# Orders of ScalarE's and VectorE's work in the first and last steps of an attention loop

## The reference

```python
# q, k, v: (4, 8, 576, 64); s: (4, 8, 576)
scores = scale * q @ k^T                                  # scale = 1/8
cum    = cumsum(max(s, 0))
scores = where(causal, -1e9, scores + minimum(-(cum[q] - cum[k]), 0))
attn   = exp(scores - max); attn /= sum(attn) + 1e-9
x      = (attn @ v), heads side by side                   # (2304, 512)
h = x @ w_in; x = (h - tanh(h)) @ w_out                   # 512 -> 2048 -> 512
h = x @ w2_in; solu = h * softmax(h); x = layernorm(solu) * g @ w2_out   # 512 -> 1024 -> 512
```

## Time and profile before

| | before |
|---|---|
| median of 3 runs | 807.65 us (807.53 to 807.90) |
| the profiled execution | 807.74 us |
| its span (first to last instruction) | 805.9 us |
| TensorE matmul busy | 796.3 us, 99% |
| ScalarE busy | 396.0 us, 49% |
| VectorE busy | 465.2 us, 58% |
| GpSimd busy | 274.3 us, 34% |

### The profile page before, as it was taken

How to read it: one execution, slowest core, us unless ns; L and a number is a source line. 1 busy time by engine, 2 the same in 40 slices (tenths; PEclk the granted TensorE clock), 3 DMA queues, 4 the chain that set the end, 5 groups by cost and what they waited for, 6 DMA issues and landing times.

```text
span 805.9 us, 14646 instructions
## 1 busy us (share of the span) xinstructions
PE 796.3 (99%) x4532; PEld 670.5 (83%) x4532; DVE 465.2 (58%) x1099; ACT 396.0 (49%) x936; POOL 274.3 (34%) x323
## 2 busy tenths in 40 slices
PE   8999999999999999999999999999999999999998
PEld 7788888888888899988888888888888888888886
DVE  5889999897954342432233222453568766666661
ACT  5999999998543232322223222442435434433342
POOL 3778877878100000000000000016553755444400
PEclk9999999999999999999999999999999999999999
DMA  6655566554523200000000000002000000000001
GB/s 174 171 151 150 143 153 161 149 144 119 159 93 103 79 1 1 1 1 1 1 0 0 0 0 0 1 1 99 6 1 0 27 27 27 26 26 13 26 13 53
DMA packets 77723, 46.40 MB, mean 58 GB/s; under 512 B 59824, under 2 KB 68144, under 8 KB 77680
## 3 DMA queue, kind: packets, MB, share of 16 engines
q1 hardware_dynamic: 75232, 45.19, 20.1%
q10 hardware_dynamic: 2448, 0.66, 0.4%
HBM read 40.97 MB, written 4.87 MB: 57 GB/s over the span
## 4 chain that ended last, share of the span: by engine, by line
PE 93%; POOL 2%; issue 2%; DVE 1%; DMA 1%; ACT 1%; POOLq 0%; DVEq 0%; ACTq 0%; SPq 0%
PE psum L1490 25%; PE psum L1477 24%; PE psum L1760 11%; PE psum L1727 11%; PE psum L1579 7%; PE psum L1612 5%; PE psum L1536 5%; PE psum L1743 2%; PE psum L1630 2%; PE psum L1554 1%; PE psum L1540 1%; DMA cum_bc<-cum_dram 1%; POOL x_lo L677 0%; ACT probs L894 0%; DMA cum_dram<-probs 0%
## 5 line engine op out<-in xcount | busy, mean ns | idle before, releaser
L1477 PE MATMUL psum<-x_hi,w1i 128*128 128x512 f32 (+1 forms) x640 | 182.1, 369 | 0.0
L1490 PE MATMUL psum<-gate_hi,w1o 128*128 128x512 f32 (+1 forms) x640 | 146.0, 370 | 0.0
L1477 PEld LDWEIGHTS psum<-x_hi,w1i 128*128 128x128 f32 x640 | 115.5, 188 | 20.5 <-DVE w1i L1129 0.4
L1490 PEld LDWEIGHTS psum<-gate_hi,w1o 128*128 128x128 f32 x640 | 112.5, 188 | 21.1
L1172 DVE TENSOR_TENSOR gate_lo<-gate,gate_hi 128x512 fp32r<-128x512 f32 (+1 forms) x80 | 53.5, 669 | 125.2 <-ACT gate_hi L869 125.2
L1477 PE MATMUL psum<-x_lo,w1i 128*128 128x512 f32 (+1 forms) x320 | 117.8, 368 | 0.0
L711 POOL TENSOR_TENSOR w2t<-stage 128x512 f32<-128x512 f32 x2 | 4.3, 2159 | 327.9 <-DVE w2x L1146 327.9
L869 ACT ACTIVATE gate_hi<-gate 128x512 fp32r<-128x512 f32 (+1 forms) x80 | 47.2, 590 | 134.9 <-PE psum L1490 126.5
L1160 DVE TENSOR_TENSOR gate<-psum,gate 128x512 f32<-128x512 f32 (+1 forms) x80 | 51.0, 638 | 95.8 <-ACT gate L856 94.3
L856 ACT ACTIVATE gate<-psum 128x512 f32<-128x512 f32 (+1 forms) x80 | 44.5, 556 | 111.7 <-PE psum L1477 90.7
L894 ACT ACTIVATE probs<-probs,neg_max 128x128 f32<-128x128 f32 (+2 forms) x144 | 83.6, 586 | 9.6 <-DVE neg_max L1205 9.6
(11 more groups left out here) (159 smaller groups left out, 1411.3 us busy)
## 6 DMA issues: line engine op xcount, KB each, us to landing
cum_bc<-cum_dram SPq DMA_DIRECT2D x16, 576.0 KB, 5.0
rden_T<-rden_dram SPq DMA_DIRECT2D x32, 144.0 KB, 3.1
out_x<-out_sb SPq DMA_DIRECT2D x18, 256.0 KB, 2.0
stage<-in_q SPq DMA_DIRECT2D x32, 128.0 KB, 2.5
v_raw<-in_v SPq DMA_DIRECT2D x32, 128.0 KB, 3.8
stage<-in_moe_w_in SPq DMA_DIRECT2D x16, 256.0 KB, 2.9
stage<-in_moe_w_out SPq DMA_DIRECT2D x16, 256.0 KB, 3.1
stage<-in_k SPq DMA_DIRECT2D x28, 128.0 KB, 2.4
```

What stands on the lines that cost most here:

```text
L1477: mm = pe.matmul(h_ps[j % 4][:, 0:wide(c)], wp[j][:, kt, :], xp[:, kt, 0:wide(c)], start=(n == 0), stop=(n == 3 * KT - 1))
L1490: mm = pe.matmul(y_ps[m][:, 0:wide(c)], wp[j][:, m * P:(m + 1) * P], gp[j % 2][:, 0:wide(c)], start=(j == 0 and wp is w1o_hi and gp is gat ...
```

## The change

In words:

- Step 0: ScalarE's third copy (k of pair 1) goes ahead of exp(0, 2), VectorE's third low part ahead of bias(0, 3). The tail's exponential of pair 0 moves from the end of step 0 into step 1.
- Step 1, ScalarE: an order of its own. A01 first, then the tail's exponential of pair 0, A2, copy 0, the denominators of pair 0, A3, copy 1, exp(0, 0), T, and the other exponentials behind it; B3 ahead of exp(1, 3). ScalarE's copy of k (`qk_copy(2)`) is left out; VectorE makes it (`k_copy`), behind A3's low part. VectorE makes A2's low part before the reciprocals.
- Step 15: ScalarE copies x's second half and T before exp(0, 2), not after it; GpSimd scales x before the last block of `first_x` and the high part of v; the denominators of pair 15 move into step 16, behind the copy of x's first half.
- The first up product waits block by block for x's high part, and for the low part only at the matmul that reads it.

```diff
--- before.py
+++ after.py
@@ -686,9 +686,12 @@
                     pool.wait_ge(w1i_hi_done, 1)
                     pool.tensor_tensor(w1i_lo[0][:, :, :], stage[0][:, 0:BANK].rearrange("p (k f) -> p k f", k=KT),
                                        w1i_hi[0][:, :, :].bitcast(F32), ALU.subtract).then_inc(w1i_first_done, 1)
+                    scale_x()
                     first_x(3)
-                v_hi()
-                scale_x()
+                    v_hi()
+                else:
+                    v_hi()
+                    scale_x()
                 v_lo()
 
             pool.wait_ge(pool_const, 11)
@@ -885,7 +888,7 @@
                             hi = act.activation(to(pT_hi), ps, ACT.Copy)
                         hi.then_inc(p_hi_done, 1)
 
-                def exp(h, t):
+                def exp(h, t, sl=sl):
 
                     if sl.runs(0):
                         pair, half, par = sl.pair(0)
@@ -939,44 +942,62 @@
                     for h in range(2):
                         exp(h, 0)
                         exp(h, 1)
-                    qk_copy(0)
-                    qk_copy(1)
+                    for n in range(3):
+                        qk_copy(n)
                     exp(0, 2)
-                    qk_copy(2)
                     exp(1, 2)
                     exp(0, 3)
                     exp(1, 3)
+                    return
+                if sl.fixed and sl.s == 1:
+
+                    p_hi("A01")
+                    exp(None, FULL, Slot(0, 0, PAIRS))
+                    p_hi("A2")
+                    qk_copy(0)
+                    denominators(Slot(0, 0, PAIRS))
+                    p_hi("A3")
+                    qk_copy(1)
+                    exp(0, 0)
+                    p_hi("T")
+                    rden_rows_copy()
+                    exp(0, 1)
+                    exp(1, 0)
+                    exp(1, 1)
+                    exp(0, 2)
+                    p_hi("B01")
+                    exp(1, 2)
+                    p_hi("B2")
+                    exp(0, 3)
+                    p_hi("B3")
+                    exp(1, 3)
                     exp(None, FULL)
+                    denominators()
                     return
-
-                second = sl.fixed and sl.s == 1
                 x_low_part(0)
+                if sl.fixed and sl.s == PAIRS:
+                    denominators(Slot((PAIRS - 1) // 2, (PAIRS - 1) % 2, PAIRS))
                 p_hi("A01")
                 exp(0, 0)
                 p_hi("A2")
-                if second:
-                    denominators(Slot(0, 0, PAIRS))
                 qk_copy(0)
                 exp(0, 1)
                 exp(1, 0)
-                if not second:
-                    exp(1, 1)
+                exp(1, 1)
                 p_hi("A3")
                 first_w1i(sl, 1)
                 qk_copy(1)
-                if second:
-                    exp(1, 1)
-                    p_hi("T")
                 rden_rows_copy()
-                exp(0, 2)
                 if sl.fixed and sl.s == PAIRS - 1:
                     x_low_part(1)
+                    p_hi("T")
+                exp(0, 2)
                 if sl.fixed and sl.s == LAST:
 
                     act.wait_ge(turned_p, UNITS * PAIRS)
                     act.wait_ge(v_split, 2 * PAIRS)
                     step(0, 0)
-                if not second:
+                if not (sl.fixed and sl.s == PAIRS - 1):
                     p_hi("T")
                 first_w1i(sl, 0)
                 first_w1i(sl, 2)
@@ -989,7 +1010,8 @@
                 exp(1, 3)
                 p_hi("B3")
                 exp(None, FULL)
-                denominators()
+                if not (sl.fixed and sl.s == PAIRS - 1):
+                    denominators()
 
             attention(act, slot)
 
@@ -1244,6 +1266,15 @@
                         dve.tensor_tensor(qkT_lo[par][:, at:at + width], qk_bank(sl, n)[:, 0:width],
                                           qkT_hi[par][:, at:at + width].bitcast(F32), ALU.subtract).then_inc(qk_lo, 1)
 
+                def k_copy():
+
+                    if sl.runs(1):
+                        pair, half, par = sl.pair(1)
+                        at, width = QK_PART[2]
+                        dve.wait_ge(turned_qk, 3 * pair + 3)
+                        dve.wait_ge(qk_lo, 3 * pair + 1)
+                        dve.tensor_copy(qk_flat[0][:, 0:width], qk_bank(sl, 2)[:, 0:width]).then_inc(qk_copied, 1)
+
                 if sl.fixed and sl.s == 0:
                     for t in (0, 1):
                         bias(0, t)
@@ -1251,10 +1282,9 @@
                         bias(1, t)
                     bias(0, 2)
                     bias(1, 2)
-                    qk_rest(0)
-                    qk_rest(1)
+                    for n in range(3):
+                        qk_rest(n)
                     bias(0, 3)
-                    qk_rest(2)
                     bias(1, 3)
                     bias(None, FULL)
                     return
@@ -1268,11 +1298,17 @@
                 p_lo("A01")
                 bias(1, 0)
                 bias(1, 1)
-                rdens()
-                p_lo("A2")
+                if sl.fixed and sl.s == 1:
+                    p_lo("A2")
+                    rdens()
+                else:
+                    rdens()
+                    p_lo("A2")
                 bias(0, 2)
                 bias(1, 2)
                 p_lo("A3")
+                if sl.fixed and sl.s == 1:
+                    k_copy()
                 first_w1i(sl, 1)
                 if sl.fixed and sl.s == LAST:
                     step(0, 0)
@@ -1472,8 +1508,13 @@
                 n = 0
                 for kt in range(KT):
                     if j == 0:
-                        pe.wait_ge(x_lo_done, KT * c + kt + 1)
+                        if weights:
+                            pe.wait_ge(x_hi_done, kt + 1)
+                        else:
+                            pe.wait_ge(x_lo_done, KT * c + kt + 1)
                     for wp, xp in ((w1i_hi, x_hi), (w1i_lo, x_hi), (w1i_hi, x_lo)):
+                        if j == 0 and weights and xp is x_lo:
+                            pe.wait_ge(x_lo_done, kt + 1)
                         mm = pe.matmul(h_ps[j % 4][:, 0:wide(c)], wp[j][:, kt, :], xp[:, kt, 0:wide(c)], start=(n == 0), stop=(n == 3 * KT - 1))
                         n += 1
                 mm.then_inc(up_done, 1)
```

## The result

The changed kernel takes 806.25 us (median of 20 runs, 805.72 to 806.90 but for one stray run of 1113.66) against 807.45 (806.89 to 807.91, 20 runs): ratio 0.9984, 95% interval 0.9977 to 0.9991. That is 1.20 us less by the medians and 1.3 by the ratio, whose interval is 0.7 to 1.9 us. The forecast was 806.5, or 1.21 us less. The change stays under 0.2%, the outcome to which the prediction gave 0.75. The profiled execution has a span of 804.6 against 805.9.

A forecast was written before the change was run, and what follows sets the result against it. TensorE was taken as the bound, so only its waits before 213 us could go: 0.63 at the start plus 0.58 at the end, 1.21 us off 807.74, gives 806.53, called 806.5; own range 806.2 to 806.9, 8-in-10 range 805.7 to 807.7.

The forecast's parts named there:

- What bounds the kernel: From 213.24 us to the end TensorE is busy 589.27 of 592.66 us; the change only moves its arrival there.
- Step 0: k's copy and low part moved ahead; step 1's scores start at about 16.93 instead of 17.35, gain 0.42 us.
- rival B: Start's gain goes, as pair 2's q and k rows aren't there or ScalarE is late; 807.2 us, chance 0.18.
- Step 1: k's transposes start at 22.04 instead of 23.09, TensorE 1.05 us early; a wait of 0.35 stays there.
- Step 2: ScalarE reaches the x copy at 29.57 instead of 30.20; only 0.63 us of the 1.05 is kept.
- Steps 15 and 16: First up product 0.21 us earlier; attention matmul at 196.75 instead of 197.33, 0.58 us early in all.
- C: Step 15's x copy is released at 188.06; the end gives only 0.3 us, total 806.8; chance 0.12.
- D: ScalarE's queue in step 1 costs 0.3 us more at each of five waits; slower, 808.1 us; chance 0.06.
- E: No effect, as waits move elsewhere by the same amount; 807.6 us; chance 0.06.
- A: Step 2's limit doesn't bite, the whole 1.05 us stays; gain 1.63, 806.1 us or a little less; chance 0.20.
- The rule weighed: If VectorE's k copy held the shared ports, GpSimd's k parts would end 0.69 us later; no such hold expected.

The follow-up runs named there:

- e3: Kernel before with only k's copy and low part moved ahead of exp(0,2) and bias(0,3) in step 0; one timed run, 807.01 us.
- e10: Changed kernel with, in step 2 alone, ScalarE's exp(1,1) behind A3, copy 1 and the reciprocals' rows copy; 806.15 us, ratio 0.9979 to the kernel before.
- e2: Kernel before with only the edits of steps 15 and 16 and of the up waits; 806.91 us, ratio 0.9991.
- e1: Kernel before with only the edits of steps 0 and 1; 806.84 us, ratio 0.9992.
- e4: Changed kernel with, in step 2 alone, ScalarE's exp(1,1) behind A3's high part; 806.11 us, ratio 0.9980 to the kernel before.
- e9: Changed kernel with the first up product waiting for each block's low part before its first matmul, as before; one timed run, 806.35 us.
- e6: Changed kernel with GpSimd's scaling of step 15 back behind x's last block and v's high part; one timed run, 807.02 us.

## Why the prediction was right, point by point

- **What bounds the kernel.** TensorE's stretch behind 211.92 us is unchanged to 0.02, so the lead at that point is the whole gain: 1.32 in the trace, 1.21 forecast.
- **Step 0.** Forecast 0.42. Nine of the twelve traces with this part show step 1's scores at 5.19 to 5.22, 0.40 to 0.43 earlier; e3 has 0.33. The changed kernel's own profile has 0.11, and e10's 0.12: there TensorE waited 0.18 (13.76 in the profile above) and 0.16 for pair 1's q, a DMA. I had looked at pair 2's rows for that (rival B), not at pair 1's, whose lateness delays k's copy and with it the scores. The trace before could have warned me: its last load of q landed at 13.55 and the transposes that read it start at 13.59. Nor is the late q clearly a price of the new order: in e2, which keeps the old one, those transposes start 0.04 later from the first bias than before (1.90, not 1.86), and the scores come 0.04 later too. How often q is late in the timed runs, no run shows.
- **Step 1.** Forecast 1.05 at k's transposes and at step 2's start, counted with step 0; e1 has (23.09 - 11.73) - (21.99 - 11.66) = 1.03 and 1.01. The wait that stays at k's transposes is given as 0.35; the prediction's own terms make it 0.63 - (1.05 - 0.62) = 0.20, and it measured 0.23. The sum does not use it. VectorE's copy of k took 0.69, as taken.
- **Step 2.** Forecast: ScalarE only 0.63 early, and TensorE with it. The mechanism was right (e10, with e4 short of it) and the size off: in e1 the x copy is 0.75 early, as ScalarE did not wait at B3, where the forecast has a wait of 0.12, and step 2 takes back 0.26, not 0.42. The start is worth 0.75 without the q wait and 0.44 with it; the forecast's 0.63 lies between them.
- **Steps 15 and 16.** Up product: forecast 0.21, measured 0.25; its release came 0.03 after the matmuls' end (187.12 to 187.15), not 0.07. Attention matmul: forecast 0.58, measured 0.68. A2's three transposes took 0.24, where I had taken 0.33. The cover at x's last block was 0.36 (low part done at 195.21, first read at 195.57), near the 0.4 I named for the split waits, and there was no wait; e9 shows that without the split 0.22 would be lost.
- **Rivals.** B, C, D and E did not come. Of the 0.42 that A would have kept in step 2, 0.16 stayed in e1, less 0.04 that step 1 fell short. The profiled 1.32 is 0.44 at the start, 0.68 at the end, 0.12 from the first bias that came sooner, and 0.08 elsewhere. With q in time the two ends would add up to 0.75 + 0.68 = 1.43, which is an estimate. So part of the closeness of the two numbers is luck: the q wait took 0.31, the start without it and the end gave 0.12 and 0.10 more than forecast.
- **The rule weighed.** VectorE's new copy at 22.90 ran beside GpSimd's subtraction at 23.05, which took 1.29 us and stood 0.18 behind its cast, both as in the earlier trace rows. The exclusive lock on the shared ports that the Trainium skill describes (SBUF — State Buffer, "SBUF: two separate sides") left no trace here, as the row of before had suggested.

## What to carry to other kernels

When one engine is the bound, add up its waits, then ask of each what is next late, and carry every engine's own lead forward: in e1 TensorE won 1.01 us by the end of step 1 and the kernel kept 0.75, as ScalarE's lead in the next step was 0.75. A wait whose release has two conditions is won only when both come early (e4 against e10, and e6, where 0.25 already won was lost behind a scaling not moved). And count distances from the event that a DMA sets: two executions differed by 0.5 us at the first bias, more than most of the parts were worth.

## What the runs showed of the hardware

The time at which the DMAs at the start land scatters: `cum_bc`, 576 KB, issued at 7.28 to 7.66 us, landed at 10.92 to 11.58, and with it the first bias moved by half a microsecond (11.25 to 11.80). The second load of pair 1's q, 128 KB, issued at 9.47 to 9.86, landed at 12.22 to 12.57 in six of the fourteen traces and at 13.13 to 13.71 in the other eight. In those eight the transposes that read it start 0.04 to 0.07 behind the landing, and in two of them TensorE shows a wait for it (0.18 and 0.16).

The rest was as read from the trace before: between steps 3 and 15, twelve steps came out within 0.13 us of each other in fourteen traces.
